# A gated attention and mixture-of-experts kernel on one core: scores, carried state and update laid out per head on halves of TensorE's array

## The reference

```python
for t in range(S):
    kt, vt, qt = (k[:, :, t], v[:, :, t], q[:, :, t])
    m_new = np.maximum(f_gate[:, :, t] + m, i_gate[:, :, t])
    f_stab = np.exp(f_gate[:, :, t] + m - m_new)
    i_stab = np.exp(i_gate[:, :, t] - m_new)
    m = m_new
    C = f_stab[:, :, None, None] * C + i_stab[:, :, None, None] * np.einsum('bhd,bhe->bhde', vt, kt)
    n = f_stab[:, :, None] * n + i_stab[:, :, None] * kt
    h_tilde = np.einsum('bhde,bhe->bhd', C, qt)
    nq = np.einsum('bhd,bhd->bh', n, qt)[:, :, None]
    denom = np.maximum(np.abs(nq), 1.0)
    o = 1.0 / (1.0 + np.exp(-o_gate[:, :, t]))
    y[:, :, t] = o * h_tilde / denom
```

## Time and profile before

| what | us |
|---|---|
| median of 3 runs | 823.14 (821.55 to 823.72) |
| profiled execution, its device time | 826.35 |
| its span in the trace | 824.6 |
| attention stage, first scores to the last step | about 12 to 177 |
| routing of the first expert, first weights | about 177 to 228 |
| eight experts and the shared network | about 228 to 819 |

### The profile page before, as it was taken

One profiled execution on the slowest core, in us unless ns is written; L12 is line 12 of the kernel. 1 busy time (PEld: TensorE's weight loads), 2 busy tenths in 40 slices (PEclk: granted clock), 3 DMA queues, 4 the chain that ended last, 5 costly groups with the idle time before them and its releaser, 6 DMA issues.

```text
span 824.6 us, 17035 instructions
## 1 busy us (share of the span) xinstructions
PE 767.3 (93%) x5535; PEld 719.1 (87%) x5535; DVE 585.4 (71%) x1454; ACT 323.3 (39%) x775; POOL 166.5 (20%) x244
## 2 busy tenths in 40 slices
PE   4999999984299999999999999999999999999995
PEld 3999999973188998899899889989998998999995
DVE  5766777766767886887787778768867886884442
ACT  4655666620213441452345135323613441352331
POOL 7356777510100011021001101100110110011001
PEclk9989999975589999999999999999999999999998
DMA  7787888510500410140041005003100400230000
GB/s 162 194 227 202 235 219 220 141 39 2 169 1 1 141 29 25 33 138 24 0 140 29 24 0 169 24 0 115 54 24 0 149 27 16 67 101 25 1 1 24
DMA packets 73407, 65.78 MB, mean 80 GB/s; under 512 B 35232, under 2 KB 64544, under 8 KB 73376
## 3 DMA queue, kind: packets, MB, share of 16 engines
q1 hardware_dynamic: 63584, 51.94, 22.7%
q0 software_dynamic: 2688, 8.65, 3.3%
q10 hardware_dynamic: 7104, 4.79, 1.8%
HBM read 56.71 MB, written 8.65 MB: 79 GB/s over the span
## 4 chain that ended last, share of the span: by engine, by line
PE 87%; DVE 8%; issue 2%; DMA 1%; ACT 1%; SPq 0%; POOL 0%; ACTq 0%; DVEq 0%
PE bank L825 19%; PE bank L827 17%; PE bank L826 17%; PE bank L668 6%; PE bank L715 5%; PE bank L843 4%; PE bank L844 4%; PE bank L703 2%; PE bank L696 2%; PE bank L679 2%; PE bank L749 1%; PE bank L660 1%; PE bank L868 1%; PE bank L869 1%; DMA s<-w 1%
## 5 line engine op out<-in xcount | busy, mean ns | idle before, releaser
L825 PE MATMUL bank<-wo_hi,h_hi 128*128 128x320 f32 x384 | 120.8, 315 | 0.0
L827 PE MATMUL bank<-wo_hi,h_lo 128*128 128x320 f32 x384 | 118.7, 309 | 0.0
L826 PE MATMUL bank<-wo_lo,h_hi 128*128 128x320 f32 x384 | 118.0, 307 | 0.0
L1484 DVE SCALAR_TENSOR_TENSOR g_act<-g_neg,rest_alpha,bank 128x384 f32<-128x384 f32 x128 | 78.6, 614 | 44.5 <-ACT g_neg L1058 43.5
L592 POOL DMA_INDIRECT xe<-x_rows,idx_in x24 | 24.4, 1015 | 407.0 <-DVE idx_in L1424 355.5
L1058 ACT ACTIVATE g_neg<-bank 128x384 f32<-128x384 f32 x128 | 62.8, 491 | 101.6 <-PE bank L844 101.6
L1056 ACT ACTIVATE h_hi<-bank 128x384 fp32r<-128x384 f32 x64 | 31.5, 491 | 170.4 <-PE bank L844 170.4
L1062 ACT CAST h_hi<-g_act 128x384 fp32r<-128x384 f32 x128 | 65.6, 512 | 79.5 <-DVE g_act L1484 79.0
L825 PE MATMUL bank<-yT_hi,wi_hi 128*128 128x384 f32 x256 | 92.3, 361 | 0.3 <-DVE yT_lo L1510 0.3
L827 PE MATMUL bank<-yT_hi,wi_lo 128*128 128x384 f32 x256 | 86.7, 339 | 0.0
L826 PE MATMUL bank<-yT_lo,wi_hi 128*128 128x384 f32 x256 | 86.7, 339 | 0.0
(11 more groups left out here) (229 smaller groups left out, 1834.2 us busy)
## 6 DMA issues: line engine op xcount, KB each, us to landing
s<-w SPq DMA_DIRECT2D x8, 1280.0 KB, 9.3
s<-w SPq DMA_DIRECT2D x8, 1024.0 KB, 5.2
s<-w SPq DMA_DIRECT2D x16, 256.0 KB, 6.2
k_in<-kT SPq DMA_DIRECT2D x24, 160.0 KB
q_wide<-qT SPq DMA_DIRECT2D x48, 80.0 KB
k_row<-k SPq DMA_DIRECT2D x24, 160.0 KB, 3.3
v_in<-v SPq DMA_DIRECT2D x24, 160.0 KB, 3.8
gate_o<-o SPq DMA_DIRECT2D x24, 160.0 KB, 3.0
```

Source lines behind the costliest of these rows:

```text
L825: pe.matmul(acc, ah, bh, start=start, stop=False, skip_group_check=True)
L826: pe.matmul(acc, ah, bl, start=False, stop=False, skip_group_check=True)
L827: return pe.matmul(acc, al, bh, start=False, stop=stop, skip_group_check=True)
L1484: dve.scalar_tensor_tensor(out=g_act[:, n, :], in0=g_neg[:, :], scalar=rest_alpha[:, j:j + 1], in1=acc, op0=ALU.mult, op1=ALU.add).then_in ...
```

## The change

Each head gets one half of the 128 rows: heads with u = 0 rows 0 to 39, heads with u = 1 rows 64 to 103, for y = 0 to 3. Scores are 8 matmuls of 64 rows and 128 moving columns instead of 4 of 128 rows and 256 columns; those of the two halves alternate and write to banks 2 and 3. The carried part is 8 matmuls of 64 rows and 41 columns instead of 4 of 82; those with u = 0 write to bank 4, those with u = 1 to bank 5, behind the update. The update is 8 matmuls with 40-column weights instead of 4 with 128-column weights; their outputs lie in rows 0 to 39 and 64 to 103. `state` has no zero blocks any more, `own_half` is gone, and `q_in` serves scores and carried part, so q is loaded once. The wait for `state_ready` stands ahead of the carried part, since half of that goes into the update's bank.

The diff, cut to its core:

```diff
-        state = ga("state", [P, B, HP, 2 * D1])
+        state = ga("state", [P, B, HP, D1])
-        q_wide = ga("q_wide", [P, B, 2, HP, P])
-        own_half = ga("own_half", [PD, 2])
...
+        CARRIED = [CARRY[:, 0:HP * D1], UPD[:, HP * D1:2 * HP * D1]]
+        UPDATE = UPD[:, 0:HP * D1]
...
-                sp.dma_start(k_in[0:PD, b, :, :], kT[c, b].rearrange("u d y s -> (u d) y s")).then_inc(qk_in[b], 16)
-                for half in range(2):
-                    sp.dma_start(q_wide[D * half:D * half + D, b, half, :, :], qT[c, b, half]).then_inc(qk_in[b], 16)
+                for u in range(2):
+                    sp.dma_start(k_in[ROWS * u:ROWS * u + D, b, :, :], kT[c, b, u]).then_inc(qk_in[b], 16)
+                for u in range(2):
+                    sp.dma_start(q_in[ROWS * u:ROWS * u + D, b, :, :], qT[c, b, u]).then_inc(qk_in[b], 16)
...
-                    for half in range(2):
-                        sp.dma_start(q_in[D * half:D * half + D, b, :, :].rearrange("d (a u) s -> d a u s", u=2),
-                                     qT[c, b].rearrange("u d (a n) s -> n d a u s", n=2)[half]).then_inc(q_rows_in[b], 16)
...
-            pool.memset(q_in[:, :, :, :], 0.0)
-            pool.memset(state[:, :, :, :], 0.0)
...
                 for y in range(HP):
-                    ins = pe.matmul(SCORE[y // 2][:, 2 * P * (y % 2):2 * P * (y % 2) + 2 * P], k_in[:, b, y, :],
-                                    q_wide[:, b, :, y, :], start=True, stop=True)
+                    for u in range(2):
+                        ins = pe.matmul(SCORE[u][:, P * y:P * y + P], k_in[half_rows(u), b, y, :], q_in[half_rows(u), b, y, :],
+                                        start=True, stop=True)
...
+                if not first(T, 1) and (not isinstance(T, int) or T <= NT - B):
+                    pe.wait_ge(state_ready, T)
...
-                    pe.matmul(pair(CARRY[:, 0:H * D1].rearrange("p (h d) -> p h d", d=D1), y), q_in[:, b, y, :], state[:, b, y, :], start=True, stop=True)
+                    for u in range(2):
+                        pe.matmul(CARRIED[u][:, D1 * y:D1 * y + D1], q_in[half_rows(u), b, y, :], state[half_rows(u), b, y, :],
+                                  start=True, stop=True)
...
-                    pe.matmul(UPD[:, 2 * D1 * y:2 * D1 * (y + 1)], k_row[:, b, 2 * D * (y // 2 + 2 * (y % 2)):2 * D * (y // 2 + 2 * (y % 2)) + P],
-                              pair(vw[:, n, :, :], y), start=True, stop=True)
+                    for u in range(2):
+                        pe.matmul(UPDATE[ROWS * u:ROWS * u + D, D1 * y:D1 * y + D1], k_row[:, b, D * (HP * u + y):D * (HP * u + y) + D],
+                                  vw[:, n, head(u, y), :], start=True, stop=True)
...
-                    ch.link(dve.tensor_tensor(carried[:, :, :], grid(CARRY), bc(gT[:, c, hs], D1), ALU.mult))
+                    for u in range(2):
+                        ins = dve.tensor_tensor(of_half(carried[:, :, :], u), CARRIED[u].rearrange("p (y d) -> p y d", d=D1),
+                                                of_half(bc(gT[:, c, hs], D1), u), ALU.mult)
...
-                            ins = dve.scalar_tensor_tensor(out=state[0:PD, b, :, cols], in0=new, scalar=own_half[:, half:half + 1],
-                                                           in1=fstate[:, n, :, cols], op0=ALU.mult, op1=ALU.add)
+                        ins = dve.tensor_tensor(state[:, b, :, :], new, fstate[:, n, :, :], ALU.add)
```

More of the change, by code:

```diff
@@ L272, in build_program @@
         gates_ready = sem("gates_ready")
-        q_rows_in = [sem(f"q_rows_in{b}") for b in range(B)]
         qk_in = [sem(f"qk_in{b}") for b in range(B)]
@@ L353, in bh_rows, with half_rows, head, of_half @@
             return slice(HB * (c % 4), HB * (c % 4) + HB)
+        def half_rows(u):
+            return slice(ROWS * u, ROWS * u + ROWS)
+        def head(u, y):
+            return 2 * y + u
+        def of_half(heads, u):
+            return heads.rearrange("p (y u) d -> p u y d", u=2)[:, u, :, :]
         def bc(ap, n):
@@ L482, in _ @@
                 pool.memset(k_in[:, b, :, :], 0.0)
-                pool.memset(q_wide[:, b, :, :, :], 0.0).then_inc(wide_zero, 1)
-            pool.memset(q_in[:, :, :, :], 0.0)
-            pool.memset(state[:, :, :, :], 0.0)
[L486 to L493, removed]
+                pool.memset(q_in[:, b, :, :], 0.0).then_inc(wide_zero, 1)
+            ch.link(pool.memset(half_ones[:, :, :], 0.0))
+            pool.memset(half_ones[:, 0, half_rows(0)], 1.0)
+            pool.memset(half_ones[:, 1, half_rows(1)], 1.0).then_inc(consts, 1)
             ch.link(pool.memset(ones_bf[:, :], 1.0))
@@ L550, in weigh_values @@
                 pool.wait_ge(state_ready, T - 1)
-                pool.tensor_tensor(fstate[:, n, :, :], state[0:PD, b, :, :], bc(fade[:, c, b, :], 2 * D1),
+                pool.tensor_tensor(fstate[:, n, :, :], state[:, b, :, :], bc(fade[:, c, b, :], D1),
                                    ALU.mult).then_inc(faded, 1)
@@ L658, in front @@
                     for y in range(HP):
-                        h = H * b + HP * half + y
+                        h = H * b + head(half, y)
                         ins = pe.matmul(LOGD[half][:, P * y:P * y + P], sel3[:, h:h + 1].to_broadcast([P, P]),
@@ L713, in back @@
                     for y in range(HP):
-                        h = HP * half + y
+                        h = head(half, y)
                         ins = pe.matmul(YB[:, D1 * h:D1 * h + D1], probs[:, n, half, y, :], v_in[:, b, h, :], start=True, stop=True)
@@ L1095, in _ @@
             dve.memset(k_in[:, 0, :, :], 0.0)
-            dve.memset(q_wide[:, 0, :, :, :], 0.0).then_inc(wide_zero0, 1)
+            dve.memset(q_in[:, 0, :, :], 0.0).then_inc(wide_zero0, 1)
+            ones_done.mark(dve.memset(UPDATE, 0.0))
             ones_done.mark(dve.memset(peak3[3 * HB:P, :], 0.0))
@@ L1226, in make_x @@
                 n = b % 2
-                ch = Chain(dve, dve_step, STEP_LINKS * T - (T if first(T, B) else B))
+                ch = Chain(dve, dve_step, STEP_LINKS * T - 2 * (T if first(T, B) else B))
                 hs = slice(H * b, H * b + H)
@@ L1242, in make_x @@
                         dve.wait_ge(faded, T - B + 1)
-                    if first(T, 1):
-                        dve.wait_ge(consts, 4)
-                    for half in range(2):
-                        cols = slice(D1 * half, D1 * half + D1)
-                        new = UPD[0:PD, 0:H * D1].rearrange("p (y d) -> p y d", y=HP)[:, :, cols]
-                        if first(T, B):
-                            ins = dve.tensor_scalar(state[0:PD, b, :, cols], new, own_half[:, half:half + 1], None, ALU.mult)
-                        else:
-                            ins = dve.scalar_tensor_tensor(out=state[0:PD, b, :, cols], in0=new, scalar=own_half[:, half:half + 1],
-                                                           in1=fstate[:, n, :, cols], op0=ALU.mult, op1=ALU.add)
+                    new = UPDATE.rearrange("p (y d) -> p y d", d=D1)
+                    if first(T, B):
+                        ins = dve.tensor_copy(state[:, b, :, :], new)
+                    else:
+                        ins = dve.tensor_tensor(state[:, b, :, :], new, fstate[:, n, :, :], ALU.add)
                     ins.then_inc(state_ready, 1)
@@ L1265, in make_x @@
                                          op0=ALU.add, op1=ALU.mult).then_inc(x_ready, 1)
-                assert ch.n == STEP_LINKS - first(T, B), ch.n
+                assert ch.n == STEP_LINKS - 2 * first(T, B), ch.n
             def step(c, b):
```

38 lines of the change are left out of this document (16 added, 22 removed).

## The result

The changed kernel takes 874.73 us in the median (865.15 to 876.14) against 822.62 (821.55 to 823.72) for the kernel before: 1.060 times as long, 95% interval 1.054 to 1.066. The direction is the forecast one, but 874.7 lies above the range of 801 to 866. The profiled execution of after took 876.04, its span 874.3.

A forecast was written before the change was run, and what follows sets the result against it. TensorE was taken to bound each attention step, with weight loads setting the pace. Middle terms -9 + 10 - 6 + 8.6 - 2.9 = +1, plus 8 clock falls of 1.7, gave +14.6 and 838 us, range 801 to 866.

The forecast's parts named there:

- Bound and pace: Attention step: TensorE waits for nobody; below some 128 columns the weight load sets the pace, 0.10 to 0.11 us each.
- Scores: Score matmuls per step: 1.35 to 1.45 us against 1.78, between full and no overlap; -18.5 to 0 in all, middle -9.
- Carried state: 16 carried matmuls instead of 8: 0.90 to 1.79 us a step against 0.85; +1 to +19 in all, middle +10.
- Update: 16 update matmuls with 40-column loads: 0.6 us a step, -6 in all, bounds -12 to +4.5.
- Changes of the division: Switches between row halves, column halves and full array: three a step at 0.13 us, +8.6 in all (0 to +10).
- State ready, other engines: Wait for the state just covered, 2 us in all without cover; VectorE allows steps of 5.95, no less; others give room.
- Start: Kernel start: the long first cast of 3.58 us shrinks as zeroing goes or shrinks, -2.9 us (0 to -3.2).
- Sum at a kept clock: All terms at the clock of now: full overlap -18 us, middle +1, no overlap +19.
- Rival A: Attention stage: halves overlap and the clock stays; 805 us with full overlap, 814 with three quarters; chance 0.33.
- The clock: TensorE clock in the attention stage: more falls to 1.2 GHz at 1.7 us each, 8 more than now.
- Rival B: Attention stage: full overlap, scores too short to restore the clock, half the work at 1.2 GHz; 859 us, chance 0.15.
- the forecast: Whole kernel: middle overlap (+1) plus 8 more clock falls, +14.6 us, 838 us; own range 825 to 848, chance 0.35.

The follow-up runs named there:

- experiment 5: Changed kernel with outputs streaming 123 columns and all scores of one row half ahead of the other's: 813.99 us, ratio 0.988 to the kernel before.
- experiment 6: Kernel before with only its scores changed: half the columns on full rows, 816.41 us; or 16 matmuls on row halves, 821.94 us.
- experiment 9: Changed kernel with the carried state's 16 matmuls streaming 82 columns instead of 41: 816.90 us, ratio 0.991 to the kernel before.
- experiment 1: Changed kernel with each output matmul streaming its 41 columns three times (123): 803.53 us, ratio 0.975 to the kernel before.
- experiment 4: Changed kernel with scores of one half after the other's, each score matmul reading all 128 rows: 834.34 us, ratio 1.012 to the kernel before.
- 8: Changed kernel with 82 columns instead of 41 in the outputs, 801.64 us; or with 123 instead of 41 in the carried state, 806.26 us.
- 3: Changed kernel with all scores of one row half ahead of the other's: 915.69 us, ratio 1.108 to the kernel before.
- experiment 7: Kernel before with the carried state's matmuls streaming 41 columns instead of 82: 825.10 us, ratio 1.005 to the kernel before.

## Why the prediction was wrong

**Bound and pace: right.** TensorE still sets the step, it waited for nothing from 36 to 158 in after, and the load sets the pace: 41 or 123 columns in the outputs make 1.81 or 1.88.

**Scores: middle wrong.** I took 1.35 to 1.45, the middle between the ends. It is 1.09, which is 8 pairs at 0.11 and one change of the division. The halves work side by side in load and in stream, so the full overlap (0.90) was the right end. In turn they would have taken not 1.79 but 1.64 (94.81 to 96.45 in experiment 5), with the change and the first carried matmuls in it: what hung on the overlap was 0.44 a step, not the 0.88 between my ends.

**Carried state: the same.** Middle +10, measured 0.82 to 0.94 for 16 against 0.85: -1 to +2. Both row terms fell at the full-overlap end, as they share one cause; I had them at a middle that no row supported.

**Update: right in sign, too small.** 0.6 expected, 0.44 measured, -9 in all instead of -6, inside the bounds.

**Changes of the division: right in size.** I had three of 0.13, 0.39 a step. Experiment 6 has 1.05 for the unchanged carried matmuls behind half-row scores against 0.85, 0.20 for a change; the router 0.77 against 0.61, 0.16; ahead of the scores 1.09 against 0.89 for 8 pairs at 0.11, 0.20. In after a step has the one ahead of the scores and the one ahead of the router, 0.36; the one from the carried state to the update lies within the update's 0.44.

**State ready, other engines: right, next to nothing.** No wait for the state shows in after; with 82 columns in the outputs, where the clock is held, it ends three waits of the carried matmuls, 0.7 us in all. That VectorE allows steps of 5.95, "no less", was too high a floor: experiment 9 has one of 5.84. **Start: right**, 2.6 of 2.9.

**Sum at a kept clock.** Full overlap gave -18 and 805 (Rival A); with the clock held by other means the changed geometry takes 801.6 to 803.5, some 20 under the kernel before. My middle of +1 was 20 too high, and it hid part of the error in the clock: the step below is off by more than the total.

**The clock: the step that failed.** The direction and the cause were right: no idle gap, but matmuls with few columns, and shorter scores, take it away. (The clock rose at 67.1, 1.3 us into the scores that start at 65.79, and not behind them.) The size was not. I priced a fall at 1.7 us, the only one that the earlier trace rows show, and took 8 of them, 13.6 us, as if falls were separate events that the next scores end. In after they do not end them: some 17 of 24 steps run at 1.2 GHz (the balance above), and what the clock costs is 71 us (experiment 1) in place of the 13.6. Rival B had the right mechanism (full overlap, scores too short to bring the clock back) but half the stage's work for 54 us where it was about three quarters, and only 0.15 of the chance. Beside that I weighed the overlap and the clock as separate terms. They are not separate: the shorter scores alone gave back in clock some 10 of the 12 us that they saved (experiment 6), and together with the narrower carried and update matmuls the stage stays at 1.2 GHz. The scores alone (experiment 6) come to -2 in all, all but the scores (experiment 4) to +11, together +52: 43 more than their sum. No term taken by itself from the profile of before could show that; that its clock was already falling, in its stretch with the fewest columns, was the sign that the kernel stood near an edge.

**Where Rival A and the forecast stood.** I had named a step under 6.2 us at full clock as what would refute the forecast: it takes 5.84. That A did not come about is the clock alone. TensorE was busy 122.00 of 122.00 us while its granted clock averaged 0.58. The page "TensorE: Matmul & The Clock Gate" of the Trainium skill, section "Why this matters for your kernels", blames idle gaps between bursts of matmuls; that does not explain this loss, and with no gap the time would be, as an estimate, the sum at full overlap, 805. The rule of the page "TensorEngine Tiling" of the Trainium skill, section "Key Properties", that different tiles load and multiply in parallel, is what the traces show: 16 scores in 1.09, where 13 in turn take 1.30. Its other rule, that a change of the mode drains the engine, also agrees, with 0.16 to 0.20 a change.

**What stays open.** How the chip decides is not settled. The runs show that more columns bring the clock back, in whatever matmul and in pairs of halves as on full rows (experiments 1, 8, 9), and that as many columns on 64 rows at a time do not hold it where those on 128 do (3 against 4). Whether the measure is rows times columns, the array's power or something else, they do not tell apart. The change's update was not tried alone, so its share of the +11 in experiment 4 is not known; half the columns in the carried state cost 1 to 7 us in the mean where the rest was as before (experiment 7). Why one kernel takes different times from one execution to the next (experiments 6 and 7) is open, too.

## What to carry to other kernels

Before shortening TensorE's work, look at the granted clock of the stretch: if it falls at all while the engine is busy, a change that packs the same work into fewer or narrower streams can lose at once more than it saves, and its terms do not add. Where loads set the pace, columns are nearly free (here up to 123, 1.88 against 1.81): let narrow matmuls stream copies into unused or overwritten columns, and measure that first. And when two terms hang on one unknown (here: do row halves overlap), give both the same end, not a middle each.

## What the runs showed of the hardware

- Matmuls on two row halves, issued alternately, run side by side in load and in stream: 8 pairs with 128 columns take 1.09 together with a change of the division, 8 pairs with 41 columns 0.82 to 0.94; 16 on column halves with 40-column loads take 0.44.
- The halves need not be issued in turn for that: with all scores of one half ahead of the other's, the trace starts carried matmuls of the first half between the last scores of the second, 0.11 to 0.12 for each such pair.
- A change between row halves, column halves and the full array costs 0.16 to 0.20 us.
- The clock can stay at 1.2 GHz for tens of microseconds with the engine busy without a gap (53.89 to 91.40), return for 3.4 and fall again. At 1.2 GHz the pieces of a step take 1.6 to 1.9 times as long.
- 82 instead of 41 columns in 16 of the 81 matmuls of a step, at no cost in their own time (1.85 against 1.81), changed the whole kernel's time by 8%, by way of the clock (0.99 instead of 0.58 from 36 to 158).
